# Value sums written beside the first keys, and the first ten tiles ranked ahead of the last two

## The reference

```python
# 1. attention, 8 heads of 64: a window of 15 keys to either side, and one summary per block of 32
k_sum = k.reshape(B, H, nb, 32, D).max(axis=3)
v_sum = v.reshape(B, H, nb, 32, D).mean(axis=3)
a = softmax([mask(scale * q @ k.T), scale * q @ k_sum.T + log(32)])
x = a @ [v, v_sum]
# 2. mixture of 8 experts, two for each token
noisy = x @ w_gate + log1p(exp(x @ w_noise)) * noise
top2 = the two largest of 8, with their softmax as weights
x = sum over the two of weight * relu(x @ w1[e]) @ w2[e]
# 3. mixture of 8 experts, at most one for each token
x = x + (x @ w_skip > 0) * p[argmax] * relu(x @ w1[e]) @ w2[e]
```

## Time and profile before

| what | value |
|---|---|
| median of three runs | 670.94 us |
| time of the profiled execution | 678.62 us |
| its span, first to last instruction | 676.1 us |
| TensorE busy | 625.1 us, 92% of the span |
| VectorE, ScalarE, GpSimd busy | 54%, 44%, 35% |
| mean granted TensorE clock | 0.957 |
| matrix products of the two mixtures in the chain that ended last | L843, L837 and L951: 62% |

### The profile page before, as it was taken

One profiled execution on the slowest core, in us unless ns is written; L12 is line 12 of the kernel. 1 busy time (PEld: TensorE's weight loads), 2 busy tenths in 40 slices (PEclk: granted clock), 3 DMA queues, 4 the chain that ended last, 5 costly groups with the idle time before them and its releaser, 6 DMA issues.

```text
span 676.1 us, 13586 instructions
## 1 busy us (share of the span) xinstructions
PE 625.1 (92%) x4071; PEld 557.6 (82%) x4071; DVE 364.5 (54%) x712; ACT 297.0 (44%) x538; POOL 234.5 (35%) x221
## 2 busy tenths in 40 slices
PE   6798863999999999999999999999699999999994
PEld 5577761799999999999999999996478888788883
DVE  4667739354644536454463545431675577556641
ACT  1667824143433434343343444324264576545531
POOL 2557102300725528072462706406023123231130
PEclk9999955899999999999999999999699999999998
DMA  9999931551572927448292654887196759567321
GB/s 318 342 282 265 306 144 52 177 188 63 141 207 54 273 61 187 124 120 231 53 255 74 174 147 89 223 297 165 20 328 221 231 191 343 162 201 249 63 47 16
DMA packets 57634, 119.81 MB, mean 177 GB/s; under 512 B 13588, under 2 KB 13972, under 8 KB 57568
## 3 DMA queue, kind: packets, MB, share of 16 engines
q1 hardware_dynamic: 39424, 94.59, 42.7%
q0 software_dynamic: 14304, 23.93, 16.9%
q10 hardware_dynamic: 3840, 0.49, 0.4%
HBM read 103.51 MB, written 23.50 MB: 188 GB/s over the span
## 4 chain that ended last, share of the span: by engine, by line
PE 82%; DVE 6%; DMA 5%; issue 3%; ACT 1%; POOLq 0%; POOL 0%; DVEq 0%; SPq 0%; ACTq 0%
PE bank L843 22%; PE bank L837 21%; PE bank L951 19%; PE bank L826 2%; DMA xg<-x_moe,ix_take 2%; PE bank L806 2%; PE bank L733 2%; PE bank L745 2%; PE bank L685 2%; PE bank L705 2%; PE bank L716 2%; PE bank L967 1%; DMA out<-y_sb,ix_put 1%; PE bank L755 1%; PE bank L667 1%
## 5 line engine op out<-in xcount | busy, mean ns | idle before, releaser
L1580 DVE TENSOR_TENSOR w_lo<-stage,w_hi x120 | 141.6, 1222 | 22.8 <-ACT w_hi L1076 18.7
L1076 ACT CAST w_hi<-stage x120 | 119.7, 1050 | 9.0 <-PE bank L951 8.9
L843 PE MATMUL bank<-unit_hi,w_hi 128*128 128x416 f32 x256 | 92.6, 362 | 0.0
L837 PE MATMUL bank<-tok_hi,w_hi 128*128 128x416 f32 x256 | 90.5, 354 | 0.6 <-DVE tok_lo L1790 0.6
L1185 ACT ACTIVATE unit_hi<-bank 128x416 fp32r<-128x416 f32 x64 | 33.2, 519 | 129.8 <-PE bank L837 117.2
L843 PE MATMUL bank<-unit_lo,w_hi 128*128 128x416 f32 x256 | 90.1, 352 | 0.0
L1838 DVE SCALAR_TENSOR_TENSOR unit_lo<-bank,unit_hi 128x416 fp32r<-128x416 f32 x64 | 37.9, 592 | 96.7 <-ACT unit_hi L1185 71.8
L837 PE MATMUL bank<-tok_hi,w_lo 128*128 128x416 f32 x256 | 89.7, 351 | 0.0
L843 PE MATMUL bank<-unit_hi,w_lo 128*128 128x416 f32 x256 | 89.7, 350 | 0.0
L1394 POOL DMA_INDIRECT x_more<-more_out,ix_put x32 | 52.1, 1627 | 42.1 <-DVE more_out L1809 26.3
L1406 POOL DMA_INDIRECT x_moe<-rows_out,ix_put x32 | 55.3, 1727 | 9.8 <-issue 9.8
(11 more groups left out here) (163 smaller groups left out, 1080.7 us busy)
## 6 DMA issues: line engine op xcount, KB each, us to landing
stage<-in_moe_w SPq DMA_DIRECT2D x128, 512.0 KB, 5.4
v_win<-in_v SPq DMA_DIRECT2D x24, 198.0 KB, 9.1
v_raw<-in_v SPq DMA_DIRECT2D x6, 528.0 KB, 13.4
x_moe<-rows_out SPq DMA_DIRECT2D x12, 260.0 KB, 4.0
kt<-in_k SPq DMA_DIRECT2D x8, 384.0 KB, 9.8
q_ring<-in_q SPq DMA_DIRECT2D x6, 512.0 KB, 10.2
x_att<-x_sb POOLq DMA_DIRECT2D x12, 256.0 KB, 5.5
x_part<-x_moe SPq DMA_DIRECT2D x4, 768.0 KB, 8.1
```

The costliest lines, as they stand in the source:

```text
L837: last = eng.matmul(ps_unit[f % 2][:, 0:W], w, x, start=(i == 0), stop=(i == len(mine) - 1))
L843: last = eng.matmul(ps_out[chunk][:, 0:W], w[:, WC // 2 + f, chunk * P:(chunk + 1) * P], h[:, f % UNITS, :], start=(f == 0 and i == 0), st ...
L1076: eng.copy(piece(w_hi[n % SETS], j), stage[:, j, :]).then_inc(s_hi, 1)
L1580: eng.tensor_tensor(piece(w_lo[n % SETS], j), stage[:, j, :], piece(w_hi[n % SETS], j).bitcast(F32), ALU.subtract)\
```

## The change

- Job "v" stands ahead of `turn_p` on PE and ahead of `empty_pt` on ACT. vsum is no tensor of its own any more: it is rows 0 to 23 of the value window 0 (batch 0) or 4 (batch 1), so ACT writes the first window itself, and POOL copies it beside the seven others.
- POOL copies the keys of both windows of a tile first and the maxima after both. DVE makes the maxima of batch 1 at turns 3 (two), 4 and 5.
- SP issues the queries and keys of batch 0 and 1 one tile earlier and the constants of the casts one tile later; DVE's four casts move from turn 2 to 9. ACT issues four small loads only after the keys of batch 0 have landed.
- The 8 filling transposes at turn 2, and the 8 at turn 27, are left out.
- POOL rounds all 8 pieces of expert 0 (at tiles 5 to 11), and DVE splits all 8 in the attention, at turns 13, 15, 17, 19, 21, 23, 24, 25.
- The router products of the last two tiles go to bank 0 (ps_gate_tail). Tile 10 is transposed ahead of the last `times_v` and multiplied behind it. The noise scale and the best two of tiles 0 to 9 are made while PE works at tile 11; those of tiles 10 and 11 follow.
- `keep_warm(11)` before the first gathered rows instead of 12, and it does not wait any more for DVE's four memsets (s_last_gates).

```diff
+        TAIL = 2
+        ps_gate_tail = bank[0]
...
-        vsum = [sb_in(att, f"vsum{b}", [NSUM, VROW]) for b in range(BATCH)]
+        vsum = [v_win[0:NSUM, b * NWIN % WR] for b in range(BATCH)]
...
-        KEY_MAXIMA = {4: (0,), 5: (1,), 6: (2,), 7: (3,)}
+        KEY_MAXIMA = {3: (0, 1), 4: (2,), 5: (3,)}
...
             elif job[0] == "v":
+                if job[1]:
+                    eng.wait_ge(s_pv, NG * ((job[1] * NWIN - WR) // 2 + 1))
...
-            eng.dma_start(c_early[:, casts - early:], const[:, casts:]).then_inc(s_casts, 16)
...
-                if t == 1:
+                if t == 0:
                     load_queries(1)
                     load_keys(1)
+                elif t == 1:
+                    eng.dma_start(c_early[:, casts - early:], const[:, casts:]).then_inc(s_casts, 16)
...
-            IDLE = {0: 16, 1: 8, 2: 8, STEPS + 3: 8}
+            IDLE = {0: 16, 1: 8}
...
-                eng.wait_ge(s_x, t + 1 if t < NT - 2 else NT)
+                eng.wait_ge(s_x, t + 1)
                 cols = 2 * E
+                ps, at = (ps_gate, t) if t < NT - TAIL else (ps_gate_tail, t - (NT - TAIL))
...
                 eng.wait_ge(s_first, PIECES // 2)
-                eng.wait_ge(s_last_gates, 2)
-                keep_warm(12, ps_turn)
+                keep_warm(11, ps_turn)
                 for t in range(PARTS):
                     eng.wait_ge(s_take[t], 16)
                     turn_x(0, t, ps_first[t])
                     keep_warm(0 if t == PARTS - 2 else 3, ps_turn)
+                eng.wait_ge(s_last_gates, 2)
...
                 if s < STEPS and s % NG == 0:
                     scores(s // NG)
+                for job in at_step.get(s, []):
+                    if job[0] == "v":
+                        do_job(job)
                 if 0 <= s - TURN_LAG < STEPS:
                     turn_p(s - TURN_LAG)
...
+                if s - PV_LAG == STEPS - 1:
+                    do_job(("x", NT - 2))
                 if 0 <= s - PV_LAG < STEPS:
                     times_v(s - PV_LAG)
+                if s == STEPS + PV_LAG:
+                    wait_job(eng, ("x", NT - 2))
+                    router_logits(NT - 2)
...
+            eng.wait_ge(s_k[0, PAIRS - 1], 16)
             eng.dma_start(c_late[:, P:early], const[:, P:early]).then_inc(s_late, 16)
...
-            ROUND_AT = (20, 22, 24, 26)
...
+                    if job == ("x", NT - 1):
+                        eng.wait_ge(s_x, NT)
+                        noise_scale(0, NT - TAIL)
+                    if job[0] == "x":
+                        empty_job(eng, job)
             eng.wait_ge(s_gt[0], NT)
+            noise_scale(NT - TAIL, NT)
...
+            def keys_of_tile(t):
+                for w in (2 * t, 2 * t + 1):
+                    window_of_keys(w)
+                for w in (2 * t, 2 * t + 1):
+                    if w % NWIN < WKR:
+                        maxima_beside(w)
...
+            ROUND = {5: (0,), 6: (1,), 7: (2,), 8: (3,), 9: (4,), 10: (5, 6), 11: (7,)}
...
-            SPLIT_AT = (17, 19, 21, 23)
+            SPLIT_AT = (13, 15, 17, 19, 21, 23, 24, 25)
...
-                if s == 2:
+                if s == 9:
                     eng.wait_ge(s_casts, 16)
...
+            best_two(0, NT - TAIL)
             for group in GROUPS[0]:
                 route(0, group)
             index_lists(0)
-            for j in range(PIECES // 2, PIECES):
-                split_first(j)
             first_mixture()
```

More of the change, by code:

```diff
@@ L378, in build @@
         s_first = sem("s_first")
-        s_fhi_down = sem("s_fhi_down")
         s_fhi = sem("s_fhi")
@@ L465, in build @@
                 at_step.setdefault(s, []).append(("x", t))
+        for s in at_step:
+            at_step[s].sort(key=lambda job: job[0])
         jobs = [j for s in range(-1, LAST + 1) for j in at_step.get(s, [])]
@@ L727, in times_v @@
                         eng.wait_ge(s_win[w % WR], 16 * (w // WR + 1))
-                        eng.wait_ge(s_vw, w // NWIN * WR + min(w % NWIN + 1, WR))
+                        if w % NWIN == 0:
+                            for hh in range(2):
+                                wait_job(eng, ("v", w // NWIN, hh))
+                        else:
+                            eng.wait_ge(s_vw, w // NWIN * (WR - 1) + min(w % NWIN, WR - 1))
                 for i in range(GH):
@@ L1016, in _ @@
                 for job in at_step.get(s, []):
-                    do_job(job)
-            for t in (NT - 2, NT - 1):
-                wait_job(eng, ("x", t))
-                router_logits(t)
+                    if job[0] == "x" and job[1] != NT - 2:
+                        do_job(job)
+            wait_job(eng, ("x", NT - 1))
+            router_logits(NT - 1)
             eng.wait_ge(s_cast, 3)
@@ L1344, in _ @@
                 for w in (2 * t, 2 * t + 1):
-                    if w % NWIN < WR:
+                    if 0 < w % NWIN < WR:
                         sums_beside(w)
-                for w in (2 * t + WKR, 2 * t + WKR + 1):
-                    if w < BATCH * NWIN:
-                        window_of_keys(w)
+                if t + WKR // 2 < NT:
+                    keys_of_tile(t + WKR // 2)
                 if t >= 2:
                     store_x(t - 2)
-                if ROUND <= t < ROUND + PIECES // 2:
-                    round_first(t - ROUND)
+                for j in ROUND.get(t, ()):
+                    round_first(j)
             for t in (NT - 2, NT - 1):
@@ L1622, in totals, with best_two @@
                 eng.sem_inc(s_counted, 1)
+            def best_two(t0, t1):
+                ps = ps_gate if t0 == 0 else ps_gate_tail
+                tiles = slice(t0, t1)
+                eng.wait_ge(s_z, 2 if t0 == 0 else 4)
+                then(eng.tensor_tensor(score[:, tiles], z_sp[:, tiles], noise_sb[:, tiles], ALU.mult))
+                then(eng.tensor_tensor(
+                    score[:, tiles],
+                    ps[:, 0:(t1 - t0) * 2 * E].rearrange("p (t e) -> p t e", t=t1 - t0)[:, :, 0:E],
+                    score[:, tiles], ALU.add))
+                for t in range(t0, t1):
+                    last = eng.max(top[:, t, :], score[:, t, 0:E])
+                then(last)
+                for t in range(t0, t1):
+                    last = eng.max_index(top_ix[:, t, :], top[:, t, :], score[:, t, 0:E])
             def route(m, group):
@@ L1630, in route @@
                 if m == 0:
-                    eng.wait_ge(s_z, 2)
-                    then(eng.tensor_tensor(score[:, tiles], z_sp[:, tiles], noise_sb[:, tiles],
-                                           ALU.mult))
-                    then(eng.tensor_tensor(
-                        score[:, tiles],
-                        ps_gate[:, 0:NT * 2 * E].rearrange("p (t e) -> p t e", t=NT)[:, tiles, 0:E],
-                        score[:, tiles], ALU.add))
+                    best_two(NT - TAIL, NT)
                     ranked = score
@@ L1645, in route @@
                     ranked = logit2
-                if m == 0:
-                    for t in range(t0, t1):
-                        last = eng.max(top[:, t, :], ranked[:, t, 0:E])
-                    then(last)
-                    for t in range(t0, t1):
-                        last = eng.max_index(top_ix[:, t, :], top[:, t, :], ranked[:, t, 0:E])
-                else:
+                if m == 1:
                     then(eng.tensor_reduce(top[:, tiles, 0], ranked[:, tiles, 0:E], AX.X, ALU.max))
```

47 lines of the change are left out of this document (21 added, 26 removed).

## The result

The changed kernel takes 665.90 us (median of 20 runs, 661.57 to 670.28), the kernel before, run beside it, 673.53 us (20 runs, 670.56 to 679.51). The ratio is 0.9886 with a 95% interval of 0.9860 to 0.9912: 7.6 us faster where 12.7 were forecast. Against the 658.2 us of the prediction 7.7 us are missing. Of these, 2.6 are the baseline: the three runs shown had a median of 670.94, and all 20 have 673.53. The other 5.1 are gain that did not come.

The account below looks back on a forecast made before the run. PE, busy 92% of the span, bounds the kernel, so only an earlier first mixture product gains: 3.3 + 0 + 0.8 + 0 + 2.3 + 6.3 = 12.7 us off 670.94 gives 658.2 us, range 654.5 to 664.5.

Parts of the forecast that it names:

- Start of the attention: From the keys of batch 0 through early tiles: a shorter chain gains 3.3 us, bounds 0.9 and 3.3.
- what follows keeps up: Behind the first value sums: DVE's idle 4.74 us takes moved maxima, one 0.9 us maximum leaves the chain, PE then sets pace.
- The first half of the term: Attention start up to the first `times_v`: earlier copies and sums and no filling transposes gain 2.4 us.
- the start gives nothing: Attention start: DVE waits for the keys of batch 1 at turn 3, giving 660.6 us; chance 0.10.
- DVE has room for the four casts at turn 9: Attention, turn 9: DVE is idle there for longer than the casts' 0.9 us, while PE sets the pitch.
- The gap and the end: Before the mixture, earlier heating and faster gathers gain 6.3 us; at the attention's end, moving ACT's rounding to POOL gains 0.8.
- The middle: Mid-attention tiles: two more slowed by splits lose 0.7, a PE loss may not recur; taken as 0, bounds +0.7 and -0.5.
- The second rival: Gap before the mixture: gathers are slow by themselves, long issues stay at 2.06 and 1.94, giving 660.2 us; chance 0.13.
- Ranking: After the attention: best eight of ten tiles found beside PE's work at tile 11, gaining 2.3 us.
- that rival: Gap before the mixture: clock not up when the first product comes, 1.5 to 2 us lost, 660 us; chance 0.12.
- The one of a fall within the attention: Attention: clock falls early and stays low, about 3.6 us per tile, 687 us if at tile 4; chance 0.07.
- The mixtures: Both mixtures: a rival that they lose what the front gives, something other than PE's start setting their end, 671 us; chance 0.05.

Follow-up runs that it names:

- start_only: Kernel before with only the new start of the attention (loads, sums, maxima, no fillings at turn 2): 672.95 us, ratio 0.9997 to the kernel before.
- before_again: The kernel before, unchanged, timed against itself and profiled a second time: 673.01 us, ratio 0.9994.
- block_sums: Changed kernel, but POOL adds each of batch 1's three blocks of values when it lands: 665.89 us, ratio 0.9881 to the kernel before.
- less_8: Changed kernel without the eight filling transposes of turn 1: 664.10 us, ratio 0.9861 to the kernel before; 663.82 us, again 0.9861, when repeated.
- after_again: The changed kernel, unchanged, run once more: 664.50 us, ratio 0.9878 to the kernel before.
- values_next: Changed kernel with the value products of batch 1 one turn later in TensorE's order: 668.93 us, ratio 0.9950 to the kernel before.
- gap_only: Kernel before with only POOL's eight roundings, DVE's eight splits in the attention and heating freed of its wait: 667.07 us, ratio 0.9916 to the kernel before.
- loads_later: Changed kernel with last four splits behind the index lists and expert 1's last four loads after all gathers landed: 667.46 us, ratio 0.9899 to the kernel before.
- splits_late: Changed kernel with the last four splits, and SP's loads of expert 1, back behind the index lists: 671.36 us, ratio 0.9977 to the kernel before.
- rank_only: Kernel before with only the bank of the last two tiles and the ranking made ahead: 671.34 us, ratio 0.9969 to the kernel before.
- late_pieces: Changed kernel with expert 0's piece loads one tile later, one rounding at tile 10, two at 11: 665.38 us, ratio 0.9884 to the kernel before.
- one_round: Changed kernel with POOL rounding one piece per tile, so no split meets two roundings: 664.39 us, ratio 0.9867 to the kernel before.

## Why the prediction was off

**The step that failed** is "Start of the attention", the term of 3.3 us. start_only measured 0.2. What was wrong above all is the sentence that what follows keeps up. DVE was checked for the maxima of batch 1, and there it kept up: it made both at 19.11 and did not hold softmax back. Not checked was PE's own instruction stream. In start_only 2.2 of the 3.3 us had come at tile 4, and two stalls of 0.83 and 1.39 us, at fixed places of the stream and 1.2 to 1.6 us behind an instruction packet, took them by tile 6. In the changed kernel it is POOL's sum of values that PE meets first: it began at 37.65 (35.88 in before_again), PE waited 0.94 us for it, stalled for 0.70, and tile 6 came 9.4 us after tile 5 instead of 7.7. block_sums removed the wait for the sum, and the stall grew from 0.70 to 1.39; less_8 lost little at that place and met the stall at tile 7. The waits for values and queries (1.34 and 0.52 us of idle PE) took less: behind them tile 5 still stood 2.1 us ahead of before_again. The DMAs were busy for a share of 0.97 over the first 44 us; that this made the packets late is not shown.

The first half of the term was right in the time of tile 2's scores and less so as a gain. The profile it was read from had begun 0.7 us late, so 2.4 us there are 1.4 in start_only against before_again. And the 0.9 us for the filling transposes did not all come: without them PE waits 0.98 us for POOL's part of the value sums, which they had covered (start_only; 0.58 in the changed kernel). The rival "the start gives nothing" had the size and the wrong cause: it named the keys of batch 1. That DVE has room for the four casts at turn 9 was wrong as well: beside POOL's sum they take 4.6 us in after_again instead of 0.6. There no wait of PE names it; in values_next it is 3.19 us of idle PE.

**The gap and the end**, 6.3 and 0.8 forecast, gave 5.7 together in gap_only. The gap was nearly right: issues of 1.02, rows used 2.8 us after the third issue's end where 2.4 were forecast (2.4 in loads_later), 10.4 us from `take_ix` to the first product against 9.9 forecast; measured from before_again's 15.8 it is 5.4 us. The 0.8 at the end did not come, because of the split of 2.78 us: PE's 1.39 us of waiting for ACT became 1.55 for DVE. The prediction took 1.81 for every split beside POOL's rounding, though two roundings in a row were in the diff. This is a term mis-sized. The middle, put at 0, lost 0.4: from tile 6 to tile 11 it is 26.1 us, in before_again 25.7.

**The second rival**, slow gathers whatever DVE does, is refuted. In splits_late the issues take 2.06 and 1.94 us beside the splits, in the changed kernel 1.03 and 1.01 without them. The Trainium skill, page SBUF — State Buffer, section Who interferes with whom, infers that such a tensor_tensor leaves descriptor making alone; here two issues take twice as long beside it. Not every one does: in splits_late the first issue, of which 0.9 us lie beside the splits, took 1.12 all the same, as in the changed kernel.

**Ranking**, 2.3 forecast, gave 2.1 in rank_only (0.7 to 3.6 by its interval).

**The clock.** It came back on time in the gap (by 108.4, 3.5 us after the heating began), so in the changed kernel that rival did not occur. The one of a fall within the attention argued from one row that small products do not bring the clock back. They do: in before_again after 3.4 us. Falls of 3.4 to 10.2 us begin at 17, 35, 46, 53, 68, 80 and 84 us in various traces of these kernels. Such a fall made a tile 1.5 us longer in late_pieces, and together with the stall ahead of it 3.8 in one_round and 4.6 in loads_later. They may be a large part of the spread of 1.3% between runs; that was not measured. And because the profiled execution had the longest of them, the prediction's split of what was low clock and what was work could not be made from it. It took 0 for this, between bounds of either sign, and no run here measures that term alone.

**The mixtures** kept what the front gave, apart from 2.1 us in the second routing of the profiled pair, where the clock was at 0.50 from 460 to 462.7.

In sum the missing 5.1 us are 3.1 at the start, 1.4 in gap and end, 0.2 in the ranking, and 0.4 that the three parts gave alone and not together. Each of these rests on ratios known to some 2 us, so the stalls of the traces, and not this sum, carry the account.

**Left open:** what decides when an instruction packet is asked for, and why PE resumes over 1.2 us after its end. Also what makes the clock fall. In late_pieces, less_8 and values_next it fell within 2.1 us of PE's idling for 1.5 to 3.2 us, in one_round and loads_later within 0.2 us of the end of idle times of 1.09 and 1.42; in after_again and block_sums idle times of 1.3 and 1.4 in the value products were followed by none.

## What to carry to other kernels

A chain that is shortened on the engines gains only as far as the next thing that is late by itself: follow the gain through every sum, load and instruction packet of the following stages before it is counted. Idle time of PE without a releaser is worth counting by its place in the instruction stream, over several traces. Work that is taken out may have covered a wait, and a small DVE operation moved beside a long POOL operation can take as long as that. Splits on DVE and large loads of weights both belong away from a list of indirect gathers; here they cost 1.6 and 4.3 us of a 16 us gap. And a profiled execution that lies above the median of its kernel, here by 0.8%, needs a second one beside it before stretches are compared.

## What the runs showed of the hardware that was not expected

- TensorE stalls for up to 1.95 us at fixed places of its instruction stream, behind 340, 463, 584, 708 and 828 weight loads here, without a semaphore. Work resumes 1.2 to 1.6 us after the end of an instruction packet of DMA queue 8, and where PE reaches the place later than that, as the four traces with the old start do at the 463rd load, there is no stall.
- An indirect gather's rows are used 2.4 us after the end of its issue when no weights are loaded beside it (loads_later), and 6.1 us after it when four loads of 512 KB are (splits_late).
- The issue of such a gather takes 2.06 and 1.94 us beside DVE tensor_tensors with SBUF operands, and 1.02 us without; the first of a list took 1.12 in either case.
- One 128x1024 split on DVE takes 1.22, 1.81 or 2.78 us with none, one or two POOL roundings in a row beside it.
- A 128x128 cast on DVE takes 0.22 us alone and 3.49 or 3.58 beside a POOL addition of 3.54 us.
- The granted clock falls to 0.5 for 3.4 to 10.2 us within streams of small fp32 products, at other places in other executions, and comes back without heating; in the first profile of the kernel before, it did not come back in the 11.9 us that were left of the attention.
